# First loads in three parts, bias rows on ScalarE's queue, VectorE's first work reordered, and 12 unread products ahead of the first scores, in a fused attention and two-MLP kernel

## What is computed

```python
scores = q @ k.T / sqrt(64)                        # (4, 8, 576, 576)
cum    = cumsum(maximum(s, 0), axis=-1)
scores = where(causal, -1e9, scores + minimum(-(cum[:, None] - cum[None, :]), 0))
x = softmax(scores) @ v                            # -> (2304, 512)
h = x @ w_in;  x = (h * cos(h)) @ w_out            # 512 -> 2048 -> 512
xn = x / rms(x) * rms_g
out = (silu(xn @ w_gate) * (xn @ w_val)) @ w_out   # 512 -> 1536 -> 512
```

## Time and profile before

| | |
|---|---|
| median of 3 runs | 1075.29 us (1074.92 to 1076.4) |
| the profiled execution | 1076.61 us |
| its span, first to last instruction | 1074.8 us |
| PE busy | 98% of the span |
| VectorE, ScalarE, GpSimd busy | 57%, 45%, 24% |

### The profile page before, as it was taken

How to read it: one execution, slowest core, us unless ns; L and a number is a source line. 1 busy time by engine, 2 the same in 40 slices (tenths; PEclk the granted TensorE clock), 3 DMA queues, 4 the chain that set the end, 5 groups by cost and what they waited for, 6 DMA issues and landing times.

```text
span 1074.8 us, 16583 instructions
## 1 busy us (share of the span) xinstructions
PE 1050.1 (98%) x6116; PEld 997.0 (93%) x6116; DVE 607.5 (57%) x1160; ACT 484.5 (45%) x1030; POOL 259.8 (24%) x203
## 2 busy tenths in 40 slices
PE   5999999999999999999998999999999999999997
PEld 4998999899999999999997999999999999999997
DVE  6888888698555555555668864334334334433222
ACT  5888887655554555545455522222222321322111
POOL 5898896575000000000019630000000000000000
PEclk9999999999999999999999999999999999999999
DMA  6654542143000000000014410000000000000000
GB/s 205 192 185 139 169 153 93 53 138 108 2 1 1 1 1 0 0 0 0 0 33 118 115 60 1 30 2 1 30 0 0 29 0 0 29 0 0 30 1 30
DMA packets 23369, 52.35 MB, mean 49 GB/s; under 512 B 3921, under 2 KB 3921, under 8 KB 23313
## 3 DMA queue, kind: packets, MB, share of 16 engines
q1 hardware_dynamic: 23312, 51.62, 15.4%
HBM read 46.74 MB, written 4.87 MB: 48 GB/s over the span
## 4 chain that ended last, share of the span: by engine, by line
PE 90%; DVE 6%; ACT 1%; issue 1%; DMA 1%; POOL 0%; SPq 0%; DVEq 0%; ACTq 0%; POOLq 0%
PE psum L1232 28%; PE psum L1216 15%; PE psum L1158 15%; PE psum L1258 14%; PE psum L1108 7%; PE psum L1139 5%; PE psum L1121 4%; DVE b_r L788 1%; DVE b_lo L826 1%; DVE b_r L785 1%; DVE b_g L821 1%; PE psum L1112 1%; DMA raw<-in_qkv 0%; DVE w L866 0%; DVE xT L850 0%
## 5 line engine op out<-in xcount | busy, mean ns | idle before, releaser
L1232 PE MATMUL psum<-c_x,cw 128*128 128x384 f32 x1728 | 313.3, 335 | 0.0
L1232 PEld LDWEIGHTS psum<-c_x,cw 128*128 128x128 f32 x1728 | 303.4, 188 | 6.1
L1216 PE MATMUL psum<-b_hi,w 128*128 128x384 f32 x768 | 211.5, 336 | 6.0 <-DVE b_lo L826 5.9
L1216 PEld LDWEIGHTS psum<-b_hi,w 128*128 128x128 f32 x768 | 140.1, 188 | 8.7 <-DVE b_lo L826 8.5
L927 DVE TENSOR_TENSOR c_t<-psum,c_t 128x384 f32<-128x384 f32 x72 | 40.1, 557 | 182.8 <-ACT c_t L671 182.4
L1258 PE MATMUL psum<-cw,c_hi 128*128 128x512 f32 x432 | 136.3, 396 | 1.0 <-DVE c_lo L931 0.8
L671 ACT ACTIVATE c_t<-psum 128x384 f32<-128x384 f32 x72 | 35.4, 492 | 209.5 <-PE psum L1232 208.3
L1216 PE MATMUL psum<-b_lo,w 128*128 128x384 f32 x384 | 128.3, 334 | 0.0
L1108 PE MATMUL psum<-qk 128*128 128x192 f32 (+6 forms) x480 | 99.9, 338 | 11.5 <-DVE qk L715 8.7
L1158 PE MATMUL psum<-bx_even,w 128*128 128x384 f32 x576 | 108.0, 335 | 1.5 <-DVE xT L770 1.5
L1158 PE MATMUL psum<-bx_odd,w 128*128 128x384 f32 x576 | 107.6, 334 | 0.0
(11 more groups left out here) (93 smaller groups left out, 1473.8 us busy)
## 6 DMA issues: line engine op xcount, KB each, us to landing
raw<-in_qkv SPq DMA_DIRECT2D x15, 864.0 KB, 4.4
stage<-in_w_out SPq DMA_DIRECT2D x28, 256.0 KB, 2.7
raw<-in_qkv SPq DMA_DIRECT2D x16, 320.0 KB, 3.1
inv_row<-inv_rows SPq DMA_DIRECT2D x32, 144.0 KB, 3.4
out<-stage SPq DMA_DIRECT2D x18, 256.0 KB, 2.1
cum<-cum_rows SPq DMA_DIRECT2D x30, 144.0 KB, 3.2
stage<-in_w_in SPq DMA_DIRECT2D x16, 256.0 KB, 2.7
stage<-in_w_gate SPq DMA_DIRECT2D x12, 256.0 KB, 2.7
```

Source lines behind the costliest of these rows:

```text
L1216: last = mm(Y_BANKS[f][:, 0:TB], out1_w(j, a)[:, cols], g[j % 2][:], start=(j == 0 and m == 0), stop=(j == NJ - 1 and m == 2))
L1232: last = mm(to[:, 0:TC], weights(c, a)[:, kc], c_x[:, b, kc], start=(kc == 0 and m == 0), stop=(kc == KC - 1 and m == 2))
```

## The change

The first pair's keys and queries are loaded and split in three parts instead of two (keys and tile 0; tiles 1 to 3; tiles 4 to 8), and these loads stand first on SP's queue. The two broadcast loads of `s` are issued by ScalarE instead of SP. VectorE copies the constants first, then makes the first low part, then the bias of pair 0, then the second low part; the third low part stands behind the logits of tile 0, and the clip and scan of all 32 rows (`all_cum`) behind the logits of tile 3. `load_qk(2)` waits for three low parts. Before everything else PE makes 12 products of the ones tile with itself in fp32, which nothing reads.

```diff
-FIRST_QK = SEQ + 2 * P
+FIRST_QK = [0, SEQ + P, SEQ + 4 * P, QK_COLS]
+FIRST_TILES = [0, 1, 4]
+WARM_UP = 12
...
+        first_v_loaded = sem("first_v_loaded")
...
                 if p == 2:
-                    sp.wait_ge(first_lo, 2)
+                    sp.wait_ge(first_lo, 3)
...
-            for a in range(2):
-                sp.dma_start(cum8[1][HALF_ROWS[a], :], s_h[a:a + 1, :].to_broadcast([64, SEQ])).then_inc(s_first_loaded, 16)
-            for n, (lo, hi) in enumerate(((0, FIRST_QK), (FIRST_QK, QK_COLS), (QK_COLS, PAIR_COLS))):
+            for n in range(3):
+                lo, hi = FIRST_QK[n:n + 2]
                 sp.dma_start(raw[0][:, lo:hi], qkv[0, :, lo:hi]).then_inc(first_loaded[n], 16)
+            sp.dma_start(raw[0][:, QK_COLS:PAIR_COLS], qkv[0, :, QK_COLS:PAIR_COLS]).then_inc(first_v_loaded, 16)
             sp.dma_start(s_sb[:], s_h).then_inc(s_loaded, 16)
...
+            for a in range(2):
+                act.dma_start(cum8[1][HALF_ROWS[a], :], s_h[a:a + 1, :].to_broadcast([64, SEQ])).then_inc(s_first_loaded, 16)
             act.wait_ge(consts_dve, 1)
             nc.scalar.activation(sine_start[:], ones_f[:, 0:1], ACT.Exp)
             nc.scalar.activation(half_pi[:], ones_f[:, 0:1], ACT.Copy, scale=math.pi / 2).then_inc(half_pi_ready, 1)
-            first_split_hi(0)
-            first_split_hi(1)
+            for n in range(3):
+                first_split_hi(n)
...
             dve.wait_ge(consts_dve, 2)
+            dve.wait_ge(consts_pool, CONSTS_POOL)
+            nc.vector.tensor_copy(ident_b[:], ident[:]).then_inc(consts_dve, 1)
+            for a in range(2):
+                last = nc.vector.tensor_copy(mask_b[HALF_ROWS[a], :], mask_f[HALF_ROWS[a], HALF_ROWS[a]])
+            last.then_inc(consts_dve, 1)
...
+            first_split_lo(0)
             dve.wait_ge(s_first_loaded, 32)
...
                                          ALU.mult, ALU.add).then_inc(first_cum, 1)
-            dve.wait_ge(consts_pool, CONSTS_POOL)
-            nc.vector.tensor_copy(ident_b[:], ident[:]).then_inc(consts_dve, 1)
-            for a in range(2):
-                last = nc.vector.tensor_copy(mask_b[HALF_ROWS[a], :], mask_f[HALF_ROWS[a], HALF_ROWS[a]])
-            last.then_inc(consts_dve, 1)
...
-            first_split_lo(0)
             first_split_lo(1)
-            dve.wait_ge(s_loaded, 16)
-            nc.vector.tensor_scalar(s_sb[:], s_sb[:], 0.0, 1.0 / SCORE_SCALE, ALU.max, ALU.mult).then_inc(spos_ready, 1)
-            dve.wait_ge(spos_ready, 1)
-            nc.vector.tensor_tensor_scan(cum[:], ones_f[0:NH, 0:1].to_broadcast([NH, SEQ]), s_sb[:], 0.0,
-                                         ALU.mult, ALU.add).then_inc(cum_ready, 1)
             dve.wait_ge(first_cum, 1)
+
+            def all_cum():
+
+                dve.wait_ge(s_loaded, 16)
+                nc.vector.tensor_scalar(s_sb[:], s_sb[:], 0.0, 1.0 / SCORE_SCALE, ALU.max, ALU.mult).then_inc(spos_ready, 1)
+                dve.wait_ge(spos_ready, 1)
+                nc.vector.tensor_tensor_scan(cum[:], ones_f[0:NH, 0:1].to_broadcast([NH, SEQ]), s_sb[:], 0.0,
+                                             ALU.mult, ALU.add).then_inc(cum_ready, 1)
...
                 do(0, logits, 0)
+                if t == 0:
+                    first_split_lo(2)
...
                 do(0, logits, 3)
+                if t == 0:
+                    all_cum()
                 do(0, logits, 4)
...
                 if p == 0:
-                    at_least(pool, first_loaded[2], 16)
+                    at_least(pool, first_v_loaded, 16)
...
+            pe.wait_ge(consts_dve, 1)
+            for _ in range(WARM_UP):
+                mm(bank[7][:, 0:P], ones_f[:], ones_f[:], start=True, stop=True)
             pe.wait_ge(consts_pool, CONSTS_POOL)
             pe.wait_ge(consts_dve, CONSTS_DVE)
...
-                if p == 0 and n in (0, 2):
-                    pe.wait_ge(first_lo, 1 if n == 0 else 2)
+                if p == 0 and n in FIRST_TILES:
+                    pe.wait_ge(first_lo, FIRST_TILES.index(n) + 1)
```

More of the change, by code:

```diff
@@ L480, in first_split_hi @@
             def first_split_hi(n):
-                lo, hi = ((0, FIRST_QK), (FIRST_QK, QK_COLS))[n]
+                lo, hi = FIRST_QK[n:n + 2]
                 act.wait_ge(first_loaded[n], 16)
@@ L699, in _ @@
             dve.wait_ge(consts_dve, 2)
[L700 to L704, removed]
             dve.wait_ge(consts_pool, CONSTS_POOL)
@@ L718, in _ @@
             first_split_lo(0)
-            first_split_lo(1)
-            dve.wait_ge(s_loaded, 16)
-            nc.vector.tensor_scalar(s_sb[:], s_sb[:], 0.0, 1.0 / SCORE_SCALE, ALU.max, ALU.mult).then_inc(spos_ready, 1)
-            dve.wait_ge(spos_ready, 1)
-            nc.vector.tensor_tensor_scan(cum[:], ones_f[0:NH, 0:1].to_broadcast([NH, SEQ]), s_sb[:], 0.0,
-                                         ALU.mult, ALU.add).then_inc(cum_ready, 1)
-            dve.wait_ge(first_cum, 1)
+            dve.wait_ge(s_first_loaded, 32)
+            nc.vector.tensor_scalar(cum8[1][:], cum8[1][:], 0.0, 1.0 / SCORE_SCALE, ALU.max, ALU.mult).then_inc(first_pos, 1)
+            dve.wait_ge(first_pos, 1)
+            nc.vector.tensor_tensor_scan(cum8[0][:], ones_f[:, 0:1].to_broadcast([P, SEQ]), cum8[1][:], 0.0,
+                                         ALU.mult, ALU.add).then_inc(first_cum, 1)
+            first_split_lo(1)
+            dve.wait_ge(first_cum, 1)
+            def all_cum():
[4 more added lines that the diff above has]
+                                             ALU.mult, ALU.add).then_inc(cum_ready, 1)
             def logits(p, n):
```

## The result

The changed kernel takes 1079.12 us (1078.17 to 1081.49, 7 runs) against 1075.97 us for the kernel before in the same session (1074.92 to 1076.4, 7 runs): a ratio of 1.0032, with a 95% interval of 1.0022 to 1.0042. It is slower by 0.32%, about 3.4 us, where 2.4 us of gain were forecast. The profiled execution (1080.61 us, the second slowest of the seven) spans 4.0 us more than that of before.

What follows compares the result with a forecast made beforehand. PE, busy without a gap from about 30 us, bounds the kernel. 2.9 + 1.7 - 1.8 = 2.8, some 3.0 us of gain, capped at 2.4 by pair 2's load: 1072.9 us against 1075.29, range 1071.7 to 1075.0.

Steps and rivals of the forecast that it cites:

- The first load: At the start: issued at 0.74 instead of 2.00, landing at 4.6 instead of 6.60; first logits 2.9 us earlier.
- a limit of 6.3: Broadcasts on ScalarE's queue, expected at about 5, would hold VectorE if they landed after 6.3 us.
- Warm-up and level: PE's 12 unread products take 5.2 us, raising the clock before tile 1; it must survive idling from about 7.8 to 9.5.
- the 1.7 us for tiles 1 to 3: Pair 0, tiles 1 to 3: PE at the upper clock level saves 1.7 us in all.
- Rival B: Tiles 1 to 3 lack the upper clock level, 1.7 us isn't saved, 0.7 us gain remains: 1074.6; chance 0.12.
- `all_cum`: Clip and scan between the logits of tiles 3 and 4 take 1.82 us, ending at 14.5 instead of 11.69.
- What is late next: Loads behind `cum_ready` go 2.8 us later; `load_qk(2)` at 17.3 limits the gain at pair 2 to 2.4 us.
- rival A: Pair 2's load isn't the bound, landing within 6.0 us of issue; PE keeps 3.0 us: 1072.3; chance 0.14.
- the slack of 5.3 us: At pair 2: GpSimd's low part ended at 27.0 and PE wanted it at 32.30, a slack of 5.3 us.
- The rest of the chain: From pair 2 to the end, each landmark stands 2.4 us earlier, with no further loss.
- C: At the start, broadcasts hold the first load until 6.4, leaving 0.6 us of gain: 1074.7; chance 0.16.
- D: Later loads' bytes served ahead of `load_qk(2)` add 3.3 us, making the kernel slower: 1076.2; chance 0.04.

Runs made afterwards that it cites:

- Experiment 5: Changed kernel in which GpSimd's first split (pair 1) waits until all rows are scanned; ratio to the kernel before 1.0009.
- experiment 1: Changed kernel with clip and scan of all rows back between the second low part and the first logits; ratio to the kernel before 0.9988.
- experiment 2: Kernel before with one edit only, clip and scan of all rows moved behind the logits of tile 3; ratio to the kernel before 1.0022.
- experiment 3: Changed kernel without the 12 unread products; ratio to the kernel before 1.0030.
- experiment 6: Changed kernel with the clip of all rows made by ScalarE, only the scan left behind the logits of tile 3; ratio to the kernel before 1.0015.
- experiment 7: Changed kernel with GpSimd's subtraction for pair 1 issued in two halves of 864 columns; ratio to the kernel before 1.0030.
- experiment 10: Changed kernel, rows of s loaded first, clip and scan before pair 0's bias, 16 more products after tile 0's scores; ratio to the kernel before 0.9992.
- experiment 4: Changed kernel with 14 more unread products behind the scores of tile 0; ratio to the kernel before 1.0042.
- experiment 8: Kernel of experiment 1 without the 12 unread products; ratio to the kernel before 0.9999.
- experiment 11: Kernel of experiment 10 without the 16 products behind tile 0's scores; ratio to the kernel before 0.9985.
- experiment 9: Kernel before with one edit only, the 12 unread products ahead of PE's first waits; ratio to the kernel before 0.9993.

## Why the prediction was wrong

**The first load**: right in kind. Expected at 4.6, it landed at 4.14, 2.5 us earlier than before. The earlier issue alone gives 1.25 of that, and 64 KB less at 366 GB/s 0.2, so more was won than the time of issuing. The broadcasts on ScalarE's queue paid for it: expected at about 5, they landed at 7.14, and VectorE waited 1.31 us for them. The forecast had a limit of 6.3 beyond which they would hold VectorE, and didn't price it. So the first logits came at 9.38 instead of 8.7, still 2.24 us earlier than before.

**Warm-up and level**: the products took 4.5 us of the 5.2 expected and the level rose, so tile 0's scores took 1.02 us instead of 1.78. The step "It has to survive PE's idle time from about 7.8 to 9.5" failed: the idle time was 3.23 us. It began at 7.06, since tile 0's scores were already fast, and ended at 10.29 with the later first logits; the level fell near 11.2. Of the 1.7 us for tiles 1 to 3 some 0.7 came. Rival B had this, and its place in the sum is right, but it isn't what decided.

**`all_cum`**: this is the step that failed. "1.82 us now stand between the logits of tiles 3 and 4" took two durations from a moment at which GpSimd was idle but for the last 0.4 us and put them where GpSimd reads and writes for 3.9 us. They stood for 4.49 us, 14.24 to 18.73. Experiment 5 shows the cause, since it takes the neighbour away and leaves the place: 0.45 and 1.35 us again, and 2.5 us of time. Experiments 1 and 2 show that it is this term that decides: the place taken back is worth 4.7 us, the place alone costs 2.4.

The Trainium skill has the rule ("SBUF — State Buffer", section "Who interferes with whom"): VectorE and GpSimd share one pair of ports, held exclusively for a whole instruction. A tensor-by-scalar operation in a 2-port mode needs it, an operation with two inputs in SBUF (the core's memory) needs it beside a GpSimd instruction that reads there, and whoever comes second waits. No run here shows in which mode the clip ran. The traces agree with the wait: the clip ended 0.30 to 0.32 us behind the subtraction in four kernels, however early it was issued, and the scan 1.2 us behind it in two. That page wasn't weighed in the prediction, though this is the rule that speaks against the change.

**What is late next**: the mechanism held, the size didn't. `load_qk(2)` was forecast 2.8 us later and went 7.1 later (21.62 against 14.52). GpSimd then had it at 27.39, 5.8 us after the issue and not 6.8, as rival A had it. In the changed kernel it wasn't the last to arrive, because PE itself was late by then: its clock was at 0.50 from 18 to 28. In experiments 3, 6 and 7, where the clock recovered sooner, PE did wait for GpSimd at pair 2, by 0.82, 0.62 and 1.00 us. So a late `cum_ready` can cost PE time at pair 2 too, once it uses up the slack of 5.3 us that the forecast read.

**The rest of the chain**: right. Whatever PE had lost or won at pair 2 was still there at the end, within 0.7 us, in all kernels but experiment 10: compare the two last columns of the table with 32.30 and 1074.8.

**The rivals**: B and C each ended just under the time of before. D, the slower one, was a stretched load. None took the stop by GpSimd, and the 0.04 for "slower" came from D alone. The "366 GB/s at most" under C is the rate of one stretch; the same trace has 387 from 8 to 10.

Open is how the 3.4 us divide between the stop itself (2.3 us in the clip and 0.4 in the scan) and the half-rate stretch that followed PE's idle time. The profile of one execution shows the level at 0.50 until 28 in the changed kernel and until 22 to 23 in experiments 3 and 4, whose medians are no better. What speaks against the clock as the larger part is experiment 3, whose executions all have a mean granted clock of 0.997 or 0.998, against 0.992 to 0.997 in the changed kernel, while the time is the same within the intervals.

## What to carry to other kernels

Before an instruction is moved, look at what the other engines do at its new place, not only at what it frees in its old one: a duration holds only beside the neighbours it was measured with, and a VectorE operation with two operands in the core's memory, or a plain scale or clip there, should not be put beside a long GpSimd instruction. Look also at what the move pushes aside: with the clip and scan ahead of the first logits, the third low part of pair 0 came later and was stopped instead, in experiments 1, 8, 10 and 11. Work that feeds a store and a reload is best placed where an engine waits anyway, as early as its data allow; in experiment 11 that cost nothing, though it didn't measurably beat the old place. An early rise of PE's clock brought nothing that could be told from noise, neither by itself (experiments 8 and 9) nor with PE kept at work up to tile 1 (experiment 10 against 11).

## What was not expected of the hardware

A second issuing queue made the first load land earlier (3.4 us after its issue with 288 KB of broadcasts beside it, against 4.6 behind them) and the broadcasts later (4.2 and 5.8 us after their issue, against 2.9 and 3.2). Which transfer the DMA engines served first isn't shown; only the times of landing are.

The granted clock fell at different moments around an idle time. In the changed kernel it fell about 1 us after PE had resumed work behind 3.23 us, so that the products that had ended the gap ran at the upper level first: the products of tile 1 took 0.93 us and those of tile 2, right behind, 1.35. In experiments 1, 4 and 9 it fell while PE was still idle (11.4, 16.3 and 8.8, with PE back at 11.60, 19.34 and 9.28). Nor did the length of the idle time alone decide: 2.98 us left the level up in experiment 7 (1.00 from 15 on), and 2.80 us lowered it in experiment 3 (0.50 from 19.3).
